# Attention, routed experts and a feed-forward network on one core: the first q and k taken by tile, and loads and weight splits handed to other engines

## The chip, the cores and the metric

The kernel runs on one core of a Trainium2 chip. The number that counts is the device time of one execution in microseconds, and the median of several runs is compared. The core has five engines with an instruction stream each, which run on their own and wait for one another on semaphores: PE (TensorE, matrix products and transposes), DVE (VectorE), ACT (ScalarE), POOL (GpSimd) and SP (SyncE, which here only issues DMA transfers). Sixteen DMA engines move the data.

## What is computed

Three stages follow one another. The numbers are `B, H, S, D = 4, 8, 576, 64`, so `N = B*S = 2304` tokens of `512` features, 8 experts of width 1024, and a last network of width 2048.

```python
# attention in a window of 64 keys
scores = scale * q @ k.T ; mask (0 <= rel < 64) ; attn = softmax(scores) ; x = attn @ v
# mixture of experts, two of eight for each token
noisy_logits = x @ w_gate + log1p(exp(x @ w_noise)) * noise
top2, top2_w = two largest, softmax over the two
for e in range(E): h = maximum(x[mask] @ w1[e], 0); out[mask] += top2_w * (h @ w2[e])
# feed-forward
h = x @ w_in ; g = h * clip(h + 3, 0, 6) / 6 ; return g @ w_out
```

## The kernel before, in words

**Attention** goes over 18 tiles of 128 tokens, `T` from 0 to 17. q and k come in chunks of two tiles, and PE turns them (`turn_qk`) so that features lie on partitions; each chunk is two *items* (`n`), one for each half of the heads. ACT moves the turned q out of PSUM (`move_first`), DVE the turned k (`move_second`). Then for each tile: `scores` on PE, `row_max` on DVE, `exps` on ACT, `transpose_p` on PE, `move_pt` on ACT, `times_v` on PE, `normalise` on DVE, which leaves the tile's output in `x_new`. PE turns this too (`transpose_x`), and multiplies it with the gates' weights `wgn` (`gate_parts`, `gate_sum`). All of it is pipelined over the tiles: iteration `T` of PE's stream holds the scores of tile `T+1`, the turning of item `T+3`, and the product with v of tile `T-1`.

**Routing** happens meanwhile in five lots of tiles, `LOTS = ((0, 3), (3, 4), (7, 4), (11, 3), (14, 4))`. For a lot, DVE works out which two experts each token goes to and its row in the sorted copy of x; the rows stand in `slot_cur`. POOL then copies `x_new` away (`keep_x`, into `x_cur`) and scatters each tile twice to the DRAM tensor `x_sorted` with an indirect DMA (`scatter(t, k)`). Experts start when the first three lots have been scattered: ACT waits for them and loads the first three blocks of expert 0 (`load_x`), and PE turns these (`turn_x`, line 1602). The last two lots are needed later in expert 0 only.

**Weights** are brought as fp32 chunks of 128x1024 into four `stage` buffers and split into a high and a low part, which PE takes as fp32r operands. An expert has `SCH = 8` chunks, four of w1 and four of w2. POOL makes both parts: `split_hi` (line 680) multiplies by one and rounds, `split_lo` (line 690) subtracts. For expert 0 this falls into attention, and each part is written in four pieces. The semaphore `w_ready` counts chunks; `hidden` of expert 0 wants four, and `project` of column block `c` wants `5 + c // 2`. A chunk's load waits until the chunk four before it is split.

**Queues.** SP issues nearly all loads in an order written out by hand: the first q (k by ACT), chunks 1 to 3 of q and k, v of tiles 0 to 2 between them, the gates' weights, and from then on, one iteration of PE after the other, v of tile `T+1`, the chunks of q and k, and the chunks of expert 0's weights where `FIRST_AT` says. v of one tile is four transfers of 64 KB. A chunk of q and k is four transfers, or six where `pieces` cuts a tile in two 64-row halves. Tables say after which tile POOL scatters (`SCATTER_AT`) and splits (`SPLIT_AT`). `pause` is a copy by POOL that nothing uses, between two scatters. Two parts of `y_sorted` are set to zero at `ZERO_AT`, the other two later.

Where POOL stands in line with the scatters of the third lot, tiles 7 to 10, the text is this:

```python
            c = len(SPLIT_AT)
            first_there(c)
            for n in range(2 * PIECES):
                if n < PIECES:
                    split_hi(0, c, PIECES, n, n + 1)
                else:
                    split_lo(0, c, c + 1, PIECES, n - PIECES, n - PIECES + 1)
                scatter(LOTS[FIRST_LOT][0] + n // 2, n % 2)
```

**After attention** PE works through eight experts and six groups of the last network without a wait of note.

## Time and profile before

| what | value |
|---|---|
| median of 3 runs | 1024.43 us (1023.0 to 1025.25) |
| profiled execution | 1019.22 us |
| its span | 1017.5 us |
| TensorE clock granted over the span | 0.991 of full |
| PE busy | 988.1 us, 97% of the span |
| DVE, ACT, POOL busy | 417.8, 227.7, 423.5 us |

The span is the stretch between the first and the last instruction of the profiled execution; 1.7 us of its time lie outside. Busy shares are averages over stages with different limits, so only views of one stretch tell what a change there is worth. PE is an engine in order: what a change saves ahead of the experts moves all that follows.

### The profile page before, as it was taken

How to read it: one execution, taken by the hardware profiler on the slowest of the kernel's cores; microseconds unless marked ns; L12 is line 12 of the kernel's file. 1: busy time of each engine (PE TensorE's matmuls, PEld its weight loads, DVE VectorE, ACT ScalarE, POOL GpSimd, SP SyncE). 2: the span in 40 equal slices, each digit the busy share in tenths (PEclk: the TensorE clock that was granted, in tenths of full speed). 3: DMA queues.
4: the chain of work that ended last, by engine and by line, in shares of the span. 5: the costliest groups of instructions: out<-in, count | busy, mean ns of one | idle time of the engine just before them, and what ended most of it. 6: DMA issues, size and time to landing. Idle time of an engine off the chain costs nothing.

```text
span 1017.5 us, 18019 instructions
## 1 busy us (share of the span) xinstructions
PE 988.1 (97%) x7108; PEld 877.5 (86%) x7108; DVE 417.8 (41%) x897; ACT 227.7 (22%) x537; POOL 423.5 (42%) x326
## 2 busy tenths in 40 slices
PE   7989889999999999999999999999999999999998
PEld 6777668989889898989989989999999999999997
DVE  3578764313222222213222255545445445355333
ACT  4666521111111111111111121111111211111111
POOL 3067976993855739192855729101101001000000
PEclk9999879999999999999999999999999999999999
DMA  9699876764452716263342433200101111000000
GB/s 181 128 207 247 271 258 222 246 186 150 135 185 90 230 61 208 70 180 122 125 145 86 151 106 125 64 32 21 42 31 41 41 31 41 31 1 1 32 1 31
DMA packets 125878, 115.94 MB, mean 114 GB/s; under 512 B 64912, under 2 KB 93520, under 8 KB 125808
## 3 DMA queue, kind: packets, MB, share of 16 engines
q1 hardware_dynamic: 106368, 75.36, 27.0%
q10 hardware_dynamic: 13680, 20.75, 6.0%
q0 software_dynamic: 5760, 18.88, 5.8%
q8 instruction: 47, 0.77, 0.3%
q14 instruction: 23, 0.19, 0.1%
HBM read 75.90 MB, written 39.06 MB: 113 GB/s over the span
## 4 chain that ended last, share of the span: by engine, by line
PE 81%; SPq 7%; POOL 5%; DMA 3%; issue 2%; DVE 1%; ACT 0%; ACTq 0%; POOLq 0%; DVEq 0%
PE PS L1635 20%; PE PS L1755 20%; PE PS L1739 19%; PE PS L1618 19%; SPq L500 3%; SPq L490 3%; POOL x_sorted L711 3%; PE PS L1602 1%; POOL W L690 1%; POOL W L680 1%; PE PS L1680 1%; DMA x_sorted<-zeros 1%; DMA y_sorted<-y_sb 0%; PE PS L1498 0%; DMA stage<-in_moe_w_dram 0%
## 5 line engine op out<-in xcount | busy, mean ns | idle before, releaser
L1635 PE MATMUL PS<-W,hs_room 128*128 128x512 f32 (+1 forms) x960 | 245.2, 399 | 0.1
L1618 PEld LDWEIGHTS PS<-xs,W 128*128 128x128 f32 x1536 | 231.0, 189 | 10.8 <-issue 0.2
L1618 PE MATMUL PS<-xs,W 128*128 128x256 f32 (+2 forms) x1536 | 239.7, 307 | 0.0
L1755 PE MATMUL PS<-W,gs 128*128 128x512 f32 x864 | 217.0, 396 | 0.9 <-DVE gs L1353 0.9
L1739 PE MATMUL PS<-x2s,W 128*128 128x384 f32 x1152 | 216.6, 337 | 0.0
L1739 PEld LDWEIGHTS PS<-x2s,W 128*128 128x128 f32 x1152 | 201.4, 188 | 7.2
L680 POOL TENSOR_TENSOR W<-stage,ones_f 128x1024 fp32r<-128x1024 f32 (+1 forms) x100 | 147.6, 1484 | 136.5 <-PE PS L1635 133.1
L1635 PEld LDWEIGHTS PS<-W,hs_room 128*128 128x128 f32 (+1 forms) x960 | 172.3, 186 | 34.6 <-DVE hs_room L1203 0.3
L1755 PEld LDWEIGHTS PS<-W,gs 128*128 128x128 f32 x864 | 161.5, 188 | 31.5 <-issue 1.6
L690 POOL TENSOR_TENSOR W<-stage,W 128x1024 fp32r<-128x1024 f32 (+1 forms) x100 | 185.4, 1863 | 5.8
L1203 DVE SCALAR_TENSOR_TENSOR hs_room<-PS,hs_room 128x256 fp32r<-128x256 f32 (+2 forms) x128 | 61.9, 484 | 290.6 <-ACT hs_room L899 290.6
L899 ACT ACTIVATE hs_room<-PS 128x256 fp32r<-128x256 f32 (+2 forms) x128 | 55.3, 432 | 371.0 <-PE PS L1618 354.2
L1012 ACT ACTIVATE gs<-PS 128x384 fp32r<-128x384 f32 x96 | 47.2, 492 | 307.6 <-DVE PS L1351 307.6
L787 POOL DMA_INDIRECT ya<-y_sorted,slot x18 | 17.1, 951 | 223.9 <-PE PS L1680 200.6
L1349 DVE TENSOR_SCALAR hc<-PS 128x384 f32<-128x384 f32 x96 | 53.5, 557 | 130.9 <-PE PS L1739 130.9
L1353 DVE SCALAR_TENSOR_TENSOR gs<-PS,gs 128x384 fp32r<-128x384 f32 x96 | 53.6, 558 | 60.5 <-ACT gs L1012 60.5
L1351 DVE SCALAR_TENSOR_TENSOR PS<-hc,PS 128x384 f32<-128x384 f32 x96 | 54.0, 562 | 3.3
L711 POOL DMA_INDIRECT x_sorted<-x_cur,slot_cur x36 | 35.7, 991 | 16.2 <-DVE slot_cur L1154 8.8
L834 ACT ACTIVATE probs<-PS,negmax 128x128 f32<-128x128 f32 x144 | 39.3, 400 | 2.9 <-DVE negmax L1068 2.9
L1216 DVE COPY y_sb<-PS 128x512 f32<-128x512 f32 (+1 forms) x40 | 27.0, 688 | 22.6 <-PE PS L1635 22.6
L1197 DVE TENSOR_TENSOR xs<-PS,xs 128x512 fp32r<-128x512 f32 (+1 forms) x40 | 27.1, 679 | 17.2 <-ACT xs L889 15.5
L718 POOL COPY x_cur<-x_new 128x512 f32<-128x512 f32 x18 | 10.9, 609 | 48.8 <-DVE x_new L1083 48.8
(133 smaller groups left out, 574.4 us busy)
## 6 DMA issues: line engine op xcount, KB each, us to landing
stage<-in_moe_w_dram SPq DMA_DIRECT2D x64, 512.0 KB, 4.2
x_sorted<-zeros SPq DMA_DIRECT2D x7, 1280.0 KB, 7.6
y_sorted<-y_sb ACTq DMA_DIRECT2D x33, 256.0 KB, 3.7
x_in<-x_sorted ACTq DMA_DIRECT2D x31, 256.0 KB, 4.3
vD<-in_v_dram SPq DMA_DIRECT2D x72, 64.0 KB, 2.8
out_dram<-o_sb SPq DMA_DIRECT2D x18, 256.0 KB, 2.1
stage<-in_moe_w_in_dram SPq DMA_DIRECT2D x8, 512.0 KB, 3.9
stage<-in_moe_w_out_dram SPq DMA_DIRECT2D x8, 512.0 KB, 3.8
```

Of the source, the lines that this page charges most:

```text
L680: last = nc.gpsimd.tensor_tensor(chunk_at(parity, c, 0)[:, at], stage[:, c % STAGES, at], ones_f[:].broadcast_to([P, n]), ALU.mult)
L690: last = nc.gpsimd.tensor_tensor(chunk_at(parity, c, 1)[:, at], stage[:, c % STAGES, at], chunk_at(parity, c, 0)[:, at].bitcast(F32), ALU. ...
L711: pool.indirect_dma_start(out=x_sorted, out_offset=bass.IndirectOffsetOnAxis(ap=slot_cur[:, k, t:t + 1], axis=0), in_=x_cur[:, t, :], in_o ...
L899: nc.scalar.activation(hs[:, c % 2, 0, 0:n], HP_[:, c % 2, 0:n], ACT.Relu).then_inc(hhi_done, 1)
L1203: nc.vector.scalar_tensor_tensor(hs[:, c % 2, 1, 0:n], HP_[:, c % 2, 0:n], 0.0, hs[:, c % 2, 0, 0:n].bitcast(F32), ALU.max, ALU.subtract). ...
L1349: nc.vector.tensor_scalar(hc[:, c % 2], h, 3.0, 0.0, ALU.add, ALU.max).then_inc(hc_done, 1)
L1351: nc.vector.scalar_tensor_tensor(G6[:, c % 2], hc[:, c % 2], 6.0, h, ALU.min, ALU.mult).then_inc(g6_done, 1)
L1353: nc.vector.scalar_tensor_tensor(gs[:, c % 2, 1], G6[:, c % 2], 1.0 / 6.0, gs[:, c % 2, 0].bitcast(F32), ALU.mult, ALU.subtract).then_inc( ...
L1618: last = nc.tensor.matmul(HP_[:, c % 2, 0:n], W[:, par, 0, b, at:at + P], xs[part][:, a, kd, 0:n], start=start, stop=(kd == KD - 1 and (a, ...
L1635: last = nc.tensor.matmul(Y[0:n, first + t, :], hs[:, c % 2, a, t * P:t * P + n], W[:, par, 1, b, c * DM:(c + 1) * DM], start=(c == 0 and ...
L1739: last = nc.tensor.matmul(H2P[:, c % 2, :], W[:, 0, kd // 2, b, at:at + P], x2s[par][:, a, kd, :], start=first, stop=(kd == KD - 1 and (a, ...
L1755: last = nc.tensor.matmul(OP[:, tt, :], gs[:, c % 2, a, tt * P:(tt + 1) * P], W[:, 1, c // FC, b, at:at + DM], start=(c == 0 and (a, b) == ...
```

## The change

Five things are done, in words of the diff:

1. **The first chunk by tiles.** The four transfers of q and the four of k of chunk 0 are issued tile by tile instead of by halves of the heads, and PE turns tile 0 (`turn_tile(0)`), computes its scores, and then turns tile 1. Item 2 goes into two other PSUM banks (`item_bank`). DVE's and ACT's first instructions are put in the same order.
2. **Fewer transfers on SP's queue.** v of tile 0 is issued by ACT; the two transfers of the gates' weights by POOL. Chunks 4 and 8 of q and k are no longer cut (SP itself adds what the semaphore lacks), so each of the two has four transfers instead of six.
3. **Three chunks ahead of the third lot.** `SPLIT_AT` keeps three chunks instead of five. The second lot's scatters end one iteration earlier, with pauses where splits stood. The fourth chunk is now the one that is split between the eight scatters of tiles 7 to 10, each scatter ahead of its piece, with two `keep_x` among them.
4. **The last two chunks** of expert 0 are split by ACT (`beside_hi`) and DVE (`beside_lo`) in expert 0 itself. `tables` and `places_in_y` move back by one column block.
5. **Loads and zeros.** The eighth chunk is issued at `T = 17` instead of 15, and there it waits for the fourth chunk's split. Three of the four zero stores of `y_sorted` stand behind it at `T = 17`. Ahead of the pads SP loads two chunks of expert 1 instead of four.

```diff
-    FIRST_AT = (4, 6, 8, 10, 12, 13, 14, 15)
-    SPLIT_AT = (7, 8, 11, 12, 13)
+    FIRST_AT = (4, 6, 8, 10, 12, 13, 14, 17)
+    SPLIT_AT = (7, 8, 11)
+    BESIDE = 2
...
-    ZERO_AT = (16, 17)
+    ZERO_AT = (16, 17, 17, 17)
...
-    SCATTER_AT = {8: 0, 9: 1, 10: 2, 12: 3, 13: 4, 14: 5, 15: 6}
+    SCATTER_AT = {8: (0,), 9: (1,), 10: (2,), 12: (3,), 13: (4, 5), 14: (6,)}
...
-                if c and c % 2 == 0 and r == (crossed or [0])[0]:
+                if r in crossed(c):
...
-            load_v(0)
+            load_v(1)
             load_qk(3, both)
-            load_v(1)
-            for n, w in enumerate((wg, wn)):
-                sp.dma_start(wgn[:, :, n * E:(n + 1) * E], w.rearrange("(k p) e -> p k e", p=P)).then_inc(s_small, 16)
             load_v(2)
...
-            load_expert(1, 0, QCH)
-            for n in range(len(ZERO_AT), ZERO_PARTS):
-                zero_y(n)
+            load_expert(1, 0, QCH - BESIDE)
...
+            for n, w in enumerate((wg, wn)):
+                nc.gpsimd.dma_start(wgn[:, :, n * E:(n + 1) * E], w.rearrange("(k p) e -> p k e", p=P)).then_inc(s_gates, 16)
...
-            for n in range(2 * PIECES):
+            for n in range(2 * LOTS[FIRST_LOT][1]):
+                scatter(LOTS[FIRST_LOT][0] + n // 2, n % 2)
                 if n < PIECES:
                     split_hi(0, c, PIECES, n, n + 1)
                 else:
                     split_lo(0, c, c + 1, PIECES, n - PIECES, n - PIECES + 1)
-                scatter(LOTS[FIRST_LOT][0] + n // 2, n % 2)
+                if n % 4 == 3:
+                    keep_x(kept)
+                    kept += 1
...
+            load_v_block(act, 0, 0)
             move_first(0)
+            load_v_block(act, 0, 1)
             move_first(1)
             exps(0)
+            move_pt(0, 0)
             move_first(2)
...
+            def beside_hi(c):
+                act.wait_ge(stage_full[c % STAGES], 16 * (c // STAGES + 1))
+                at = slice((c - QCH) * CH, (c - QCH + 1) * CH)
+                nc.scalar.copy(W[:, 0, 1, 0, at], stage[:, c % STAGES, :]).then_inc(beside_half, 1)
...
+            def beside_lo(c):
+
+                at = slice((c - QCH) * CH, (c - QCH + 1) * CH)
+                dve.wait_ge(w_ready, c)
+                dve.wait_ge(beside_half, c - (SCH - BESIDE) + 1)
+                nc.vector.tensor_tensor(W[:, 0, 1, 1, at], stage[:, c % STAGES, :], W[:, 0, 1, 0, at].bitcast(F32),
+                                        ALU.subtract).then_inc(w_ready, 1)
...
-            turn_qk(0)
-            turn_qk(1)
+            turn_tile(0)
             scores(0)
+            turn_tile(1)
             scores(1)
+            transpose_p(0, 0)
             turn_qk(2)
-            transpose_p(0, 0)
             turn_qk(AHEAD)
             transpose_p(0, 1)
```

On PE, at the start of the program, the rows before run from the turning of the first chunk (`q_raw`, `k_raw`) over the scores (`masks`, then `qkT`) of tiles 0 and 1 to item 2:

```order
L1422 MATMUL PS<-ident,q_raw 128x2x64 [waits raw_first0,s_ident]
L1422 MATMUL PS<-ident,q_raw 128x2x64 x3
L1422 MATMUL PS<-ident,k_raw 128x2x64 x4
L1422 MATMUL PS<-ident,q_raw 128x2x64 [waits raw_first1]
L1422 MATMUL PS<-ident,q_raw 128x2x64 x3
L1422 MATMUL PS<-ident,k_raw 128x2x64 x4
L1446 MATMUL PS<-masks,ident_b 64x512 [waits s_mask,ld_dve,ld_act]
...
L1461 MATMUL PS<-qkT 64x128 x16
L1422 MATMUL PS<-ident,q_raw 128x2x64 [waits sc_act,raw_full1]
```

The same place in the changed program, where the first tile's scores stand ahead of the second tile's turning:

```order
L1470 MATMUL PS<-ident,q_raw 128x128 [waits raw_first0,s_ident]
L1470 MATMUL PS<-ident,q_raw 128x128 x3
L1470 MATMUL PS<-ident,k_raw 128x128 x4
L1495 MATMUL PS<-masks,ident_b 64x512 [waits s_mask,ld_dve,ld_act]
...
L1470 MATMUL PS<-ident,q_raw 128x128 [waits raw_first1]
L1470 MATMUL PS<-ident,q_raw 128x128 x3
L1470 MATMUL PS<-ident,k_raw 128x128 x4
L1495 MATMUL PS<-masks,ident_b 64x512 [waits ld_dve,ld_act]
...
L1462 MATMUL PS<-ident,q_raw 128x2x64 [waits raw_full1]
```

The second wait for data has moved behind the first scores, and item 2 no longer waits for `sc_act`, the end of `exps(0)`.

On POOL, before, from the fourth chunk (in `stage_full3`) to the first scatters of tiles 7 to 10. A DMA row is a scatter, `x_cur<-x_new` is `keep_x`:

```order
L680 TENSOR_TENSOR W<-stage,ones_f 128x256 [waits stage_full3]
L680 TENSOR_TENSOR W<-stage,ones_f 128x256 x3
L711 DMA x_sorted<-x_cur,slot_cur 23552x512
L690 TENSOR_TENSOR W<-stage,W 128x256 [waits w_half]
L690 TENSOR_TENSOR W<-stage,W 128x256 x3
L718 COPY x_cur<-x_new 128x512 [waits out_moved]
L711 DMA x_sorted<-x_cur,slot_cur 23552x512
L680 TENSOR_TENSOR W<-stage,ones_f 128x256 [waits ld_full,stage_full0]
...
L680 TENSOR_TENSOR W<-stage,ones_f 128x256 [waits ld_full,stage_full1]
L711 DMA x_sorted<-x_cur,slot_cur 23552x512 [waits x_kept,slots_ready]
```

And in the changed program, from the last scatters of the second lot:

```order
L748 COPY idle<-x_cur 128x512 [waits paused]
L724 DMA x_sorted<-x_cur,slot_cur 23552x512
L724 DMA x_sorted<-x_cur,slot_cur 23552x512 [waits x_kept,slots_ready,stage_full3]
L693 TENSOR_TENSOR W<-stage,ones_f 128x256
L724 DMA x_sorted<-x_cur,slot_cur 23552x512
...
L693 TENSOR_TENSOR W<-stage,ones_f 128x256
L734 COPY x_cur<-x_new 128x512 [waits out_moved]
L724 DMA x_sorted<-x_cur,slot_cur 23552x512
L703 TENSOR_TENSOR W<-stage,W 128x256 [waits w_half]
```

Sixteen split rows (two chunks) are gone from in front of the scatter that waits for `slots_ready`, and that scatter now stands ahead of the first piece.

On SP, at the end of attention, before and then changed:

```order
L508 DMA stage<-in_moe_w_dram 128x2x512 [waits w_ready]
L500 DMA vD<-in_v_dram 64x4x64 [waits out_full,sc_full]
L500 DMA vD<-in_v_dram 64x4x64 x3
L513 DMA y_sorted<-zeros 1536x1x128
L513 DMA y_sorted<-zeros 2048x1x128 [waits sc_full]
L560 DMA stage<-in_moe_w_dram 128x1024 [waits x_loaded2,w_ready,x_loaded1,x_loaded0]
L560 DMA stage<-in_moe_w_dram 128x1024 [waits w_ready] x3
L513 DMA y_sorted<-zeros 2048x1x128 x2
```

```order
L488 DMA vD<-in_v_dram 64x4x64 [waits out_full,sc_full]
L488 DMA vD<-in_v_dram 64x4x64 x3
L530 DMA y_sorted<-zeros 1536x1x128
L525 DMA stage<-in_moe_w_dram 128x2x512 [waits w_ready,sc_full]
L530 DMA y_sorted<-zeros 2048x1x128 x3
L575 DMA stage<-in_moe_w_dram 128x1024 [waits x_loaded2,w_ready,x_loaded1,x_loaded0]
L575 DMA stage<-in_moe_w_dram 128x1024 [waits w_ready]
```

The last chunk of expert 0 has gone behind the last v, with a wait for `w_ready`, and three zero stores stand behind it.

## Rows read from the trace of the kernel before

**Rows 1.** The page: PE's clock and the DMA engines' share in 40 slices.
```profile
PEclk9999879999999999999999999999999999999999
DMA  9699876764452716263342433200101111000000
```

**Rows 2.** Windows: busy times, PEclk, DMA share, GB/s of two stretches.
```profile
60.00:104.00 44.00, 42.15 (x921) 33.10 (x919) 34.55 (x111) 30.10 (x90) 34.20 (x49) 1.00 0.97 234
...
132.00:143.00 11.00, 8.72 (x47) 7.66 (x48) 5.66 (x21) 2.87 (x5) 10.31 (x16) 0.55 0.66 220
```

**Rows 3.** Timeline of PE: start, duration, work, idle time before it and releaser.
```profile
9.66 0.41 PE L1446 MATMUL PS<-masks,ident_b 64*64 64x512 bf16 x4 [0.83 <-ACT qkT L828]
...
20.96 0.63 PE L1422 MATMUL PS<-ident,q_later 128*128 128x128 f32 x4 [0.23 <-ACT probs L834]
...
27.88 1.16 PE L1498 MATMUL PS<-vD,pT 64*64 64x65 f32 x64 [0.62 <-DMA vD<-in_v_dram]
...
45.21 0.63 PE L1422 MATMUL PS<-ident,q_later 128*128 128x128 f32 x4 [1.64 <-DMA k_later<-in_k_dram]
...
59.45 0.63 PE L1422 MATMUL PS<-ident,q_later 128*128 128x128 f32 x4 [1.99 <-DMA k_later<-in_k_dram]
```

**Rows 4.** Timeline of SP's DMA queue, 15 to 38 us.
```profile
15.01 3.48 SPq L500 DMA_DIRECT2D vD<-in_v_dram  x4
...
26.09 0.61 SPq L532 DMA_DIRECT2D wgn<-in_moe_w_gate_dram  x1
...
27.29 5.86 SPq L500 DMA_DIRECT2D vD<-in_v_dram  x8
...
33.99 3.30 SPq L490 DMA_DIRECT2D q_later<-in_q_dram  x3
```

**Rows 5.** Windows of 2 us near the start, columns as in rows 2.
```profile
12.00:14.00 2.00, 0.03 (x2) 0.00 (x0) 1.47 (x3) 1.69 (x7) 0.00 (x0) 1.00 1.36 208
```

**Rows 6.** Timeline of DVE, 105 to 131 us.
```profile
105.40 1.42 DVE L1130 TENSOR_TENSOR gap<-top_v 128x4 f32<-128x4 f32 x1
106.75 0.15 DVE L1076 TENSOR_SCALAR rsum<-PS 128x8 f32<-128x8 f32 x1
...
109.73 0.57 DVE L1139 TENSOR_TENSOR chosen_b<-hot 128x32 bf16<-128x32 f32 x1
...
113.75 0.16 DVE L1154 CAST slot_cur<-slot_f 128x8 int32<-128x8 f32 x1
...
128.85 2.35 DVE L1137 TENSOR_TENSOR hot<-iota_e,top_f 128x24 f32<-128x24 f32 x2
```

**Rows 7.** Timeline of POOL, 104 to 132 us.
```profile
104.01 2.78 POOL L690 TENSOR_TENSOR W<-stage,W 128x256 fp32r<-128x256 f32 x4
...
113.86 0.62 POOL L680 TENSOR_TENSOR W<-stage,ones_f 128x256 fp32r<-128x256 f32 x1
...
127.82 0.98 POOL L711 DMA_INDIRECT x_sorted<-x_cur,slot_cur  x1 [0.17 <-issue]
128.82 2.32 POOL L680 TENSOR_TENSOR W<-stage,ones_f 128x256 fp32r<-128x256 f32 x4
```

**Rows 8.** Timeline of PE, first block of expert 0.
```profile
134.55 1.12 PE L1602 MATMUL PS<-ident,x_in 128*128 128x128 f32 x4 [1.70 <-DMA x_in<-x_sorted]
```

**Rows 9.** Timeline of ACT, the load of expert 0's first blocks.
```profile
131.83 1.31 ACTq L864 DMA_DIRECT2D x_in<-x_sorted  x3
```

**Rows 10.** From issue to landing: the 36 scatters of line 711, then loads of x_in.
```profile
DMA to landing us min/median/max: 2.7/4.4/7.6
...
DMA to landing us min/median/max: 2.6/3.2/4.9
```

**Rows 11.** Line 1359, a low part made by DVE from a whole chunk.
```profile
L1359 DVE TENSOR_TENSOR W<-stage,W x4: 1215/1222/1255, 606.2 to 616.4; 128x1024 fp32r<-128x1024 f32 x4
```

**Rows 12.** Last two loads for expert 0 by SP, and PE's turning of them.
```profile
169.19 0.82 SPq L590 DMA_DIRECT2D x_in<-x_sorted  x2
...
173.13 1.04 PE L1602 MATMUL PS<-ident,x_in 128*128 128x128 f32 x8
```

115 lines of the change are left out of this document (68 added, 47 removed).

## The prediction, written before the changed kernel ran

> **What bounds the kernel now.** I read the slices of the page first. From about 150 us on the clock is full and PE has no gap, so nothing there can be won by other engines; the DMA engines are at four tenths or less from 430 us on [rows 1]. The change only touches the first 175 us. What it saves ahead of expert 0 moves the whole rest, one for one, and what it does not save there is lost. So the question is when PE turns the first block of expert 0: at 134.55 us [rows 8].
>
> Reading back from there by the timelines: PE waited 1.70 us for that block [rows 8]. ACT issued the load at 131.83 [rows 9], when the last scatter of the third lot had landed. POOL issued that scatter at 127.82 and ended it at 128.80 [rows 7], so landing took 3.0 us and the load 2.7. The eight scatters and eight pieces began at 113.86 [rows 7], which is when DVE had finished the rows of that lot, at 113.91 [rows 6]. So the end of attention hangs on **the slots of the third lot, plus a row of 15 us on POOL, plus 5.7 us of DMA**. The slots in turn hang on PE's and DVE's pace through the tiles.
>
> That pace: between 60 and 104 us PE is busy 42.15 of 44 us [rows 2]; it sets the pace itself. Ahead of 60 us it waits for loads three times: 0.62 us for v at 27.88, 1.64 for k at 45.21, 1.99 for k at 59.45 [rows 3]. SP's queue shows why. It issues without a gap: four v transfers in 3.48 us, eight more in 5.86, the three transfers of a cut chunk's q in 3.30 [rows 4]. Eight v transfers of 64 KB in 5.86 us are some 90 GB/s, half of what the DMA engines carry when they are full (208 GB/s at 12 us, rows 5). So SP's issuing, not the DMA engines, is what is late in the stretches of v.
>
> **The change, part by part.**
>
> *The start.* Before, scores of tile 0 begin at 9.66 [rows 3], after both halves are turned. By tile they can begin one turning and one move earlier, which I estimate at 1.6 us from the 0.63 us of four transposes [rows 3], twice, and a gap, the second turning lies under DVE's maxima, and item 2 does not wait for the exponentials. Worked through with the durations of these rows, item 4, at 20.96 before [rows 3], could start at about 18. That is 2.9 us, and the 0.62 wait for v goes too, because v of tile 1 is issued where v of tile 0 was. Together 3.5 us. But PE then runs into the loads at 45.21 and 59.45, which it already waits for. It keeps only what SP's queue gains.
>
> *SP's queue.* Four v transfers leave it: 8 in 5.86 us is 0.73 each [rows 4], so 2.6 to 2.9; I take 2.6, since part of the time is the wait of a full queue, which passes on to the next transfer. The gates' weights take 26.09 to 27.29, 1.2 us [rows 4]. The three transfers of the cut chunk's q took 3.30 us, 1.1 each [rows 4], so this is held by bandwidth too; two fewer of six save between 0 and 2.2, I take 0.6. Against that stand 256 KB of v, which ACT now issues early, right behind k, into DMA engines that are full: at 208 GB/s [rows 5] they push chunks 1 and 2 back by 1.2 us. Sum 2.6 + 1.2 + 0.6 - 1.2 = **3.2 us**, less than the 3.5 that the start could use. From both sides: nothing at all if the DMA engines set the pace, and 4.4 if the 1.2 us fill idle time. The Trainium skill, page "DMA: Bandwidth & Descriptors", section "Issuing engines are not separate DMA queues", says that DMAs of several engines run on the same 16 DMA engines, and that issuing from more than one saves the sequencer's time alone. Taken strictly, the v that moves to ACT would be worth its issue time of 2.6 only where the engines have room, and by it the sum would be 2.6 + 1.2 - 1.2 = 2.6. The trace has both stretches, full ones (rows 5) and ones with SP as the limit (rows 4).
>
> What the moved transfers cost their new queues: ACT issues two before its first move of q and two after; it sat idle there and is needed again only when PE's second turning ends. POOL issues two small ones while it has nothing else to do, about 1 us each by the scatters' 0.98 [rows 7], and PE wants the weights only behind the product with v at 27.88 [rows 3]. Both are costed at nothing; without that cover it is 2.6 us on ACT.
>
> *DVE's route to the slots.* At 105.40 a subtraction of four columns took 1.42 us, where an operation of eight columns right behind it took 0.15 [rows 6]. It ended when POOL's four low pieces of the fifth chunk, 104.01 to 106.79, ended [rows 7]. From 101 to 113 us I count five more operations of that route that took about 0.35 us over their like; the one at 109.73 with 0.57 us is the fourth of them [rows 6]. The change takes the fourth and fifth chunk off POOL there; the second lot's scatters end earlier as well, and POOL then waits for the slots. So the loss goes: 1.27 + 5 x 0.35 = 3.0 at most, nothing if PE is what DVE waits for. DVE's maxima wait for PE's scores in between, so I take two thirds, **2.1 us**. The Trainium skill, page "SBUF — State Buffer", section "SBUF: two separate sides", calls the pair of ports that VectorE and GpSimd share an exclusive lock, held for the whole instruction. The trace agrees, and more than one instruction deep: at 128.85 two small operations took 2.35 us and ended with POOL's four high pieces [rows 6, 7].
>
> *The row on POOL.* Before: 14.94 us from the first piece to the end of the last scatter. After: the last low piece (0.73) is behind the last scatter, one copy (0.6) is put between, and the first scatter cannot start before the slots, 0.3 after them. The row is **0.2 us longer** seen from the slots. Range 0 to 0.6.
>
> *The queue at the hand-over.* The eighth chunk's load waits for the fourth chunk's split, which ends 0.8 us behind the last scatter. So 0.5 MB of weights and 3 MB of zeros set off while that scatter lands and ACT loads x. Before, 1.75 MB of the zeros lay under the eight scatters, and the rest behind the load. The last scatter landed in 3.0 us and the first load in 2.7; medians are 4.4 and 3.2, maxima 7.6 and 4.9 [rows 10]. The last scatter has a head start, and x's own queue shares the engines with the zeros instead of standing behind them, so I take **1.0 us**, and for the range 0 to 6.8.
>
> *Expert 0.* DVE makes a low part of a whole chunk in 1.22 us [rows 11]; I take no more for a high part, a copy of the same size by ACT. PE needs some 4 us for a column block there (134.55 to 173.13 holds an opening and eight of them, rows 8 and 12), so both fit beside `h_hi` and `h_lo`; without that cover they would be 4.9 us. `project(4)` wants the seventh chunk, which is ready about 1 us ahead. Two things are tight: the loads of the last two blocks are issued from 169.19 to 170.01 and turned at 173.13 [rows 12], less than 1 us behind their landing; POOL's last eight scatters lie under DVE's two low parts. And two more chunks of expert 1 (1 MB) now come when expert 1's x is loaded. I take **0.6 us**, range 0 to 2.5.
>
> Sum: 3.2 + 2.1 - 0.2 - 1.0 - 0.6 = **3.5 us**. The first block of expert 0 is turned at about 130.5 instead of 134.55. The profiled execution would be 1015.7 instead of 1019.22 us. The median of the runs lies 5.2 us above the profiled one, and I take the difference over to it: 1024.4 - 3.5 = **1020.9 us**.
>
> **Rivals.** *(a) The DMA engines set the pace, not SP.* Their share is 0.97 from 60 to 104 us [rows 2]. If it is they who make PE wait at 45 and 59, the queue's relief gives 0.8 us instead of 3.2, and the kernel 3.5 - 2.4 = 1.1 us less, 1023.3. For it: the 1.1 us for a q transfer. Against: the v transfers at 90 GB/s, and the 6 in the second of the slices of 25 us [rows 1], which says that between 25 and 51 us the engines had room. Chance 0.19.
>
> *(b) Slower: zeros in front of x.* The hand-over hangs on one landing and one load. If the zeros take their full share, the scatter lands 4.6 us later and the load 2.3 (maxima against what they took). That is 6.9 us in place of 1.0, and the sum becomes 2.4 us slower, 1026.8. It decides from 4.5 us on. For it: a scatter took up to 7.6 us under such traffic. Against: the zeros are small packets on another ring. Chance 0.18 with its neighbours.
>
> *(c) More: the clock.* From 132 to 143 us PE ran at 0.55 of its clock on average [rows 2], after it had sat idle before 132 and again before 134.55. At 0.55 the 8.72 busy us hold about 4 us that full clock would not need. If PE comes to expert 0 with its clock up, up to 3 us more are won, 1018. I think it idles longer, since POOL's row gates it even more than now: PE should stand ready 4 us early. Chance 0.10.
>
> The forecast itself has 0.53. The measurement tells about 0.2%, 2 us, from no change. Faster by more takes the forecast but for its slow edge, (c), and a piece of (a): 0.62. Within 2 us: most of (a) and the edge of (b): 0.20. Slower: (b), 0.18. The range reaches from (c) with the start's 4.4, 1015.5, to just beyond (b), 1027.5.
>
> **What the profile would show.** PE's waits at 45.21 and 59.45 stay but come 3 us earlier; if they are gone, SP won more. Scores of tile 0 begin near 8 us. The slots of the third lot are ready near 108.5, with no DVE operation of 1.4 us ahead of them. The last scatter of that lot ends near 123.5. The first load of x is issued 3 to 3.5 us later and lands in 3 to 4; PE's wait ahead of its first block (line 1602 before) grows from 1.70 to about 5. If the scatter or the load takes over 6 us there, (b) is at work. Wrong altogether would be a wait of PE for `w_ready` in expert 0, or one ahead of the last two blocks or of expert 1.

## The result and the profile after

The changed kernel takes **1027.41 us** (median of 22 runs, 1023.05 to 1031.68) against 1024.68 us for the kernel before (22 runs, 1018.67 to 1028.2) on the same chip: the ratio is **1.0029, 95% interval 1.0015 to 1.0043**. It is 2.7 to 3 us slower. The forecast was 3.5 us faster.

One thing first about the profiles. The profiled execution of before, 1019.22 us, was 5.5 us under the median of its runs; that of the changed kernel, 1028.67, is 1.3 over. So the two spans (1017.5 and 1026.6) overstate the difference threefold, and what separates them from 60 to 104 us is mostly not the change, as e13 and e14 show below. Differences between kernels are taken from ratios, and the profiles are read for mechanisms.

Windows of the changed kernel, columns as in [rows 2]:
```profile
60.00:104.00 44.00, 38.77 (x848) 29.74 (x852) 30.81 (x103) 28.15 (x85) 30.88 (x43) 1.00 0.98 239
...
170.00:200.00 30.00, 27.62 (x161) 24.40 (x161) 11.00 (x30) 5.23 (x11) 25.61 (x14) 0.94 0.85 279
```
The second stretch was whole before, and this is its line there:
```profile
170.00:200.00 30.00, 29.90 (x189) 26.64 (x188) 9.37 (x18) 6.22 (x14) 29.45 (x15) 1.00 0.85 263
```
Between 170 and 200 us PE was busy all but 0.1 us, at a granted clock of 1.00. Now it idles for 2.4 us, and its clock falls to 0.94 on average.

The start, on PE's timeline, against [rows 3]:
```profile
7.47 0.41 PE L1495 MATMUL PS<-masks,ident_b 64*64 64x512 bf16 x4 [0.83 <-ACT qkT L851]
...
14.26 0.66 PE L1462 MATMUL PS<-ident,q_raw 128*128 128x128 f32 x4 [1.55 <-DMA k_raw<-in_k_dram]
...
20.93 0.66 PE L1462 MATMUL PS<-ident,q_later 128*128 128x128 f32 x4 [2.47 <-DMA k_later<-in_k_dram]
...
57.55 0.63 PE L1462 MATMUL PS<-ident,q_later 128*128 128x128 f32 x4
```
Scores of tile 0 begin at 7.47, 2.2 us earlier, and the gain is gone at 20.93, before's 20.96: PE waits for k of chunks 1 and 2. It comes back further on: the waits for k that before had at 45.21 and 59.45 are gone, and the item it turned at 59.45 is turned at 57.55. SP's queue, against [rows 4]:
```profile
16.40 3.93 SPq L488 DMA_DIRECT2D vD<-in_v_dram  x4
...
23.95 6.99 SPq L488 DMA_DIRECT2D vD<-in_v_dram  x8
31.07 1.49 SPq L565 DMA_DIRECT2D x_sorted<-zeros  x1
32.66 2.46 SPq L508 DMA_DIRECT2D q_later<-in_q_dram  x2
```
Chunk 4 is issued 1.3 us earlier (33.99 before), not 3.2: the same eight v transfers now take 6.99 us instead of 5.86.

The hand-over to expert 0, lines of POOL, SP, ACT and PE put together in order of time, against [rows 7 to 9]:
```profile
116.51 0.97 POOL L724 DMA_INDIRECT x_sorted<-x_cur,slot_cur  x1 [8.26 <-issue]
130.07 0.98 POOL L724 DMA_INDIRECT x_sorted<-x_cur,slot_cur  x1 [0.17 <-issue]
131.90 0.38 SPq L525 DMA_DIRECT2D stage<-in_moe_w_dram  x1
132.32 10.02 SPq L530 DMA_DIRECT2D y_sorted<-zeros  x3
132.90 1.90 ACTq L891 DMA_DIRECT2D x_in<-x_sorted  x3
139.10 1.11 PE L1651 MATMUL PS<-ident,x_in 128*128 128x128 f32 x4 [2.21 <-DMA x_in<-x_sorted]
```
The last transfer of the third lot ends at 131.05 and has landed at 132.90, after 1.9 us (3.0 before). The load of x issued then needs 6.2 us to reach PE (2.7 before): 0.5 MB of weights and the first of three zero stores of 1 MB were issued 1.0 and 0.6 us ahead of it. The second store was issued with it, at 132.94, and the third at 137.09.

The hand-over to expert 1, in the same way:
```profile
176.66 0.57 SPq L591 DMA_DIRECT2D x_sorted<-zeros  x1
177.28 16.99 SPq L575 DMA_DIRECT2D stage<-in_moe_w_dram  x6
183.71 1.35 ACTq L891 DMA_DIRECT2D x_in<-x_sorted  x3
189.17 1.05 PE L1651 MATMUL PS<-ident,x_in 128*128 128x128 f32 x4 [2.38 <-DMA x_in<-x_sorted]
189.87 2.91 PE L1684 MATMUL PS<-W,hs_room 128*128 128x512 f32 x6
```
The same place before:
```profile
170.78 0.57 SPq L576 DMA_DIRECT2D x_sorted<-zeros  x1
...
177.79 1.40 ACTq L864 DMA_DIRECT2D x_in<-x_sorted  x3
...
181.74 0.60 PE L1602 MATMUL PS<-ident,x_in 128*128 128x128 f32 x4
```
In the changed kernel the padding is issued at 176.66 and loads of weights follow at once, two of them into free buffers. The x load comes 7.0 us behind the padding, as before, and lands 5.5 us later; PE waits 2.38 us, and its next six matmuls take 2.91 us, where the same group took 1.56 us at 183.82. Before had no wait there. A wait of PE ahead of expert 1 is one of the three things that the prediction had named as "wrong altogether".

### The profile page after: what moved, and what is told of

Same layout as the page of the kernel before. It is cut to its first block, busy times and chain, and to the rows that moved or that the text cites. A ratio compares the mean times of both kernels' runs of the same rounds, so it can differ in the third digit from the quotient of the medians.

```text
span 1026.6 us, 18010 instructions
## 1 busy us (share of the span) xinstructions
PE 993.1 (97%) x7108; PEld 879.6 (86%) x7108; DVE 415.5 (40%) x899; ACT 230.7 (22%) x539; POOL 419.0 (41%) x315
## 4 chain that ended last, share of the span: by engine, by line
PE 83%; POOL 4%; issue 3%; DMA 3%; SPq 3%; DVE 2%; ACT 0%; POOLq 0%; DVEq 0%; ACTq 0%
PE PS L1804 19%; PE PS L1684 19%; PE PS L1788 19%; PE PS L1667 19%; POOL x_sorted L724 2%; SPq L508 2%; PE PS L1651 2%; PE PS L1547 1%; POOL W L703 1%; PE PS L1729 1%; PE PS L1526 1%; SPq L488 1%; POOL W L693 1%; DMA x_sorted<-zeros 1%; PE PS L1510 1%
## 5 line engine op out<-in xcount | busy, mean ns | idle before, releaser
L693 POOL TENSOR_TENSOR W<-stage,ones_f 128x1024 fp32r<-128x1024 f32 (+1 forms) x92 | 143.1, 1562 | 137.9 <-PE PS L1684 134.4
L703 POOL TENSOR_TENSOR W<-stage,W 128x1024 fp32r<-128x1024 f32 (+1 forms) x92 | 180.1, 1965 | 5.7
```

Source lines behind the costliest of these rows:

```text
L693: last = nc.gpsimd.tensor_tensor(chunk_at(parity, c, 0)[:, at], stage[:, c % STAGES, at], ones_f[:].broadcast_to([P, n]), ALU.mult)
L703: last = nc.gpsimd.tensor_tensor(chunk_at(parity, c, 1)[:, at], stage[:, c % STAGES, at], chunk_at(parity, c, 0)[:, at].bitcast(F32), ALU. ...
```

## The experiments

The series of runs differ in level. The kernel before had medians of 1024.5 (e1 to e4), 1019.4 (e5 to e8), 1024.1 (e9 to e12), 1019.6 (e13 to e16) and 1018.3 us (e17, e18). The second and the third series have the same chip number on record, 7, so the level isn't the chip's alone. Every ratio is to the runs of before in its own series. The ratios on record are not quotients of the two medians, and differ from them most in e3 and e10, whose medians alone would give 0.9999 and 1.0002. "Late" means behind the load that it stood ahead of.

| kernel | ratio | its series' before |
|---|---|---|
| changed | 1.0029; 1.0046; 1.0026 | 1024.7; 1024.1; 1019.6 |
| e1, e15 front part only | 0.9981; 0.9983 | 1024.5; 1019.6 |
| e7 by tile only | 1.0004 | 1019.4 |
| e2 back part only | 1.0069 | 1024.5 |
| e3, e17 zeros late | 1.0015; 1.0012 | 1024.5; 1018.3 |
| e4 expert 1's loads ahead of the padding | 1.0036 | 1024.5 |
| e10, e18 expert 1's loads late | 1.0024; 1.0008 | 1024.1; 1018.3 |
| e5, e16 both late | 0.9980; 0.9976 | 1019.4; 1019.6 |
| e6 back part only, both late | 1.0016 | 1019.4 |
| e11 both late, transfers first | 1.0007 | 1024.1 |
| e12 front part, transfers first | 1.0042 | 1024.1 |
| e8, e13 before again | 0.9997; 1.0002 | 1019.4; 1019.6 |

### e1 and e2: the two halves of the change

e1 is before with the first chunk by tile and the moves on the queues (V0 to ACT, the gates' weights to POOL, uncut chunks). e2 is before with the rest: the constants, POOL's order, the two chunks by ACT and DVE, the late loads of expert 1. In the cut below e1's lines are against the changed kernel and e2's against the kernel before.
```
 e1:  -    FIRST_AT = (4, 6, 8, 10, 12, 13, 14, 17)   e2:  +    FIRST_AT = (4, 6, 8, 10, 12, 13, 14, 17)
      +    FIRST_AT = (4, 6, 8, 10, 12, 13, 14, 15)        +    SPLIT_AT = (7, 8, 11)
           ... all of before's back part                   +    BESIDE = 2 ... all of before's start
```


> The kernel before with points 1 and 2 of the change alone (first chunk by tile, v of tile 0 by ACT, gates' weights by POOL, uncut chunks 4 and 8). Theory A, the loss is made at the hand-over and in expert 1's loads: this kernel is 0 to 2 us faster than before, and PE turns item 4 near 21 us as before, since v pushed chunk 2 back. Rival B, the start itself costs (PE idles ahead of item 4, its clock falls, later tiles find the DMA queues fuller and stall): 1 to 4 us slower, with PE's clock below 1.00 between 20 and 26 us and the turning of item 17 later than in the kernel before (102.64 us).

> The kernel before with points 3 to 5 alone (three chunks ahead of the third lot, the last two by ACT and DVE, eighth chunk and zeros at tile 17, two instead of four chunks of expert 1 ahead of the pads). Theory A: slower than before by 2 to 6 us, PE's first block of expert 0 later than 134.55 us by 0 to 4 and a wait of over 1 us ahead of expert 1's first block. Rival B: within 1 us of before or faster by up to 2, since the slots come earlier without POOL's splits.

Measured (with the 95% interval of the ratio, here and below): e1 1021.72 us, **0.9981** (0.9964 to 0.9998). e2 1032.0 us, **1.0069** (1.0046 to 1.0092). The front is a gain of 2 us and the back a loss of 7; both together are less bad than the back alone by more than the front is worth. In e2 the x load of expert 1 came late, and PE stood still for 5.45 us. Lines of SP, DVE, PE and ACT, in order of time:
```profile
176.02 0.57 SPq L580 DMA_DIRECT2D x_sorted<-zeros  x1
177.04 2.48 DVE L1303 TENSOR_TENSOR moved<-moved,blk 128x252 f32<-128x252 f32 x1
...
184.23 0.54 DVE L1219 SCALAR_TENSOR_TENSOR hs_room<-PS,hs_room 128x368 fp32r<-128x368 f32 x1
184.83 4.21 PE L1662 MATMUL PS<-W,hs_room 128*128 128x512 f32 x9 [5.45 <-DVE hs_room L1219]
...
190.93 1.39 ACTq L873 DMA_DIRECT2D x_in<-x_sorted  x3
```
From padding to load it is 14.9 us here, 7.0 in the changed kernel. What held it was DVE. ACT made a high part about 1.8 us late, behind POOL's last transfers (the last section has this), so DVE came to the nine small operations of `places_in_y` and the last routing part at 175.17, when POOL's splits had begun (174.63). They took 9.0 us. In the changed kernel they ran from 172.91 to 175.4, ahead of POOL's splits at 175.27, and took 2.5; `moved` took 0.42 us there and 2.48 here. The low part `h_lo` that PE wanted stood behind them, and ACT issues the x load behind its next high part. So a part of e2's loss is this chain and not the loads, and e6, in a series without ACT's late start, doesn't have it.

### e3 and e4: one transfer moved

e3 puts the last three stores of zeros where before had two of them, behind the first x loads. e4 loads expert 1's first four chunks ahead of the padding, as before.
```
 e3:  -    ZERO_AT = (16, 17, 17, 17)
      +    ZERO_AT = (16,)
       ...
           load_expert(1, 0, QCH - BESIDE)
      +    for n in range(len(ZERO_AT), ZERO_PARTS):
      +        zero_y(n)
 e4:  -    load_expert(1, 0, QCH - BESIDE)
      +    load_expert(1, 0, QCH)
           ... and load_expert(1, QCH) behind the padding
```


> The changed kernel with the three zero stores of tile 17 put behind expert 0's loads and the first two chunks of expert 1. Theory A: the load of expert 0's first block lands in about 3 us instead of 6.2, and the kernel is 2 to 3.5 us faster than the changed one, near before. Rival B: PE's wait for that block shrinks but the time stays within 1 us of the changed kernel, since something else (DVE's logits, the scatters) is as late.

> The changed kernel with all four w1 chunks of expert 1 loaded ahead of the pads, as before the change. Theory A: PE's wait of 2.38 us ahead of expert 1's first block and the low clock behind it go, 2 to 4 us faster than the changed kernel. Rival B: the third and fourth chunk wait for the splits of the last two chunks of expert 0, hold up the pads and the last two blocks of expert 0, and PE waits there instead: no gain or up to 4 us slower.

Measured: e3 1024.47 us, **1.0015** (0.9996 to 1.0033). e4 1027.48 us, **1.0036** (1.0022 to 1.005). In e4 the third of the four loads waits for a free buffer, which DVE's last low parts give back (21.2 us; the four take 26.7 us in SP's queue), and the padding and x of expert 0's last two blocks wait behind it: PE waits 2.38 us at 180.39 for these blocks. The wait ahead of expert 1's first block is gone (turned at 189.39); PE waits 1.19 us for DVE behind it, at 191.23. The wait has only moved. Moving loads ahead is no cure, since their buffers come free late.

### e5 and e6: both transfers late

SP also waits until expert 1's first three blocks of x have landed. e6 is e2 with the same two moves.
```
       pad(1, 1, 0)
 +     sp.wait_ge(x_loaded[PARTS[0][1] - 1], 32)
       load_expert(1, QCH - BESIDE)
```


> The changed kernel with its last three stores of zeros put late, as in e3, and in addition SP waits until the first three blocks of expert 1's x have landed before it issues the last six chunk loads of expert 1 (two of which find a free buffer at once). Theory H, the two hand-overs: beside the zeros it is the 1 MB of weights set off in front of expert 1's x that costs, PE's 2.1 us at 184.80 in e3 and the slow clock behind it, about 3.5 us in all. Then the median falls from e3's 1024.5 to about 1021 (0.9965 to 0.998 of before), x of expert 1 lands in 3 to 4 us instead of 6 to 7, and PE has no wait ahead of expert 1's first block. Theory R, the row on POOL: what is left of the loss sits ahead of 140 us, in the later slots and in DVE's maxima behind POOL's pieces. Then it stays within 1 us of e3 (1.000 to 1.0015), even if that wait is gone.

> The kernel before with points 3 to 5 of the change alone (as e2), the three stores of zeros put late and expert 1's last six chunk loads behind its x. Theory H (the two queues are all that is bad in the back part): e2's 1032.0 loses 3 for the zeros and the 5.45 us wait ahead of expert 1 with some of its slow clock, 8 us in all, 1024 (0.998 to 1.001 of before). Theory R (the row on POOL itself costs): 1027 to 1029 (1.0025 to 1.0045), with expert 0's first block turned 2 us or more later than before's 134.55.

Measured: e5 1017.17 us, **0.998** (0.9968 to 0.9992). e6 1020.2 us, **1.0016** (1.0001 to 1.0031). With both late the whole change is as good as the front part. The back part alone, with both late, is still 0.2% slow, at or just over the upper end of what theory H gave it, and its twelve runs scatter over 8 us; the reason stays open.

### e7: by tile alone

```
       load_qk(1, both)
       load_qk(2, both)
 -     load_v(1)
 +     load_v(0)
       load_qk(3, both)
 +     load_v(1)
 +     ... wgn by SP
       load_v(2)
       ... chunks 4 and 8 cut, and all of before's back part
```
The lines are against the changed kernel.


> The kernel before with q and k of the first chunk by tile, and nothing else: v of tile 0, the gates' weights and the cut chunks stay as they were, all on SP. Theory S (the prediction's: the start's gain is caught by the loads that SP issues late): PE waits at chunk 4 and 5 stay or grow by what the start won, and the median is within 1 us of before (0.999 to 1.000). Theory T (the start itself carries it): as e1, 0.998.

Measured: 1019.62 us, **1.0004** (0.9994 to 1.0014), nothing. PE's timeline shows before's waits in place:
```profile
44.98 0.63 PE L1430 MATMUL PS<-ident,q_later 128*128 128x128 f32 x4 [0.75 <-DMA k_later<-in_k_dram]
...
59.03 0.63 PE L1430 MATMUL PS<-ident,q_later 128*128 128x128 f32 x4 [1.92 <-DMA k_later<-in_k_dram]
```
So the start's own gain is caught by late loads, as forecast, and e1's 2 us come only with the moves on the queues. The moves without the start by tile were not run, so whether they need it isn't shown.

### e8, e9 and e10: before again, changed again, loads late alone

e8 and e9 change nothing. e10 is the changed kernel with e5's wait of SP and the zeros where the change has them.

> The kernel before, unchanged, as a second look. Its ratio should be 1.000 within 0.002, which gives the size of what such a comparison cannot tell. Its first profile (1019.2 us) lies 5 us under its median (1024.5); a second should lie nearer. Theory C (the stalls called issue of about 1 us inside the product with v at 72 to 76 and 94 to 103 us, which every changed kernel shows and the first profile of before does not, belong to the program): they are missing here too. Theory I (they come and go with the execution, whatever the kernel): one or both stand here, and item 17 is turned at 104 or later instead of 102.64.

> The changed kernel, unchanged, measured beside the next three and again beside the kernel before, for a profile that stands on the same footing as theirs. Its ratio to before should be 1.003 within 0.002 again. Theory I (the stalls called issue and the 4.5 us lost between 60 and 104 us come with the execution, as their absence in the last four profiles suggests): PE is busy 41 us or more of these 44. Theory C (they come with the changed program): 39 or less.

> The changed kernel with its zeros where it has them, and only the last six chunk loads of expert 1 put behind the landing of that expert's x. It completes the square: changed 1.0029, zeros late 1.0015, both late 0.998. Theory H (two costs that add up): about 0.9995, since the loads were worth 0.0035. Theory O (they overlap: with the zeros in front expert 0 starts late and the rest has slack, or the reverse): 1.001 or more. The first load of expert 0's x still lands 5.5 to 6.2 us behind its issue and PE has no wait of over 0.5 us for x of expert 1.

Measured: e8 1018.58 us, 0.9997 (0.9985 to 1.001). e9 1027.67 us, 1.0046 (1.0027 to 1.0065). e10 1024.26 us, 1.0024 (0.9997 to 1.0051), too wide to tell. Neither e8 nor e5 to e7 have stalls called issue inside the product with v from 70 to 105 us; e9 to e12 all have them. e9's PE was busy 40.1 of the 44 us, between what the two theories asked for. That left open whether the stalls go with the series; e13 to e18 bear on it.

### e11 and e12: POOL's transfers ahead of its pieces

```
 -     first_there(c)
       for n in range(2 * LOTS[FIRST_LOT][1]):
           scatter(LOTS[FIRST_LOT][0] + n // 2, n % 2)
 -         split_hi or split_lo of piece n
       ...
 +     first_there(c)
 +     split_hi(0, c, PIECES)
 +     split_lo(0, c, c + 1, PIECES)
```


> Both late, and on POOL the eight transfers of the third lot stand ahead of the fourth chunk's eight pieces instead of between them, so that the pieces lie beside the last landing and the load of x. Theory P (POOL's row sets the end of attention, as the prediction has it): eight transfers at 1.27 us take 10.2 us instead of 14.5, the last one ends near 121 instead of 125.2, and x of expert 0 could be turned 3 to 4 us earlier; PE itself is only free at 126.3, so the first block moves from 130.45 to about 127 and the kernel wins 3 us, 0.995 of before. Theory D (the DMA engines write the rows no faster than they are now sent, or chunk 4's pieces, which then end near 127.3, are waited for by the hidden layer): the landing grows by what the row shrinks, and the ratio stays at 0.998.

> The front part of the change alone (as e1, 0.998), with POOL's eight transfers of the third lot ahead of the fourth chunk's eight pieces. Theory P: 2 to 3 us less than e1, 0.995 to 0.996. Theory D: as e1. Against e11 it says what the rest of the back part (two chunks taken by ACT and DVE, one transfer pair moved) is worth once the order of the row is right: nothing by the profile so far, and then both are equal.

Measured: e11 1023.8 us, **1.0007** (0.9986 to 1.0028). e12 1027.4 us, **1.0042** (1.0019 to 1.0064). In e11 one copy, `keep_x`, still stands between the fourth and the fifth transfer; in e12 nothing does. Both theories missed. The row did shrink, to 10.4 us (115.08 to 125.47), but DVE stood still for it. DVE's timeline, and PE's behind it, in e11:
```profile
116.57 0.16 DVE L1195 TENSOR_TENSOR gate<-gap 128x4 f32<-128x4 f32 x1
125.34 0.69 DVE L1102 TENSOR_REDUCE negmax<-PS 128x4 f32<-128x512 f32 x1 [8.62 <-remote]
...
127.01 1.08 PE L1559 MATMUL PS<-ident,x_new 128*128 128x128 f32 x4 [9.12 <-DVE logits L1126]
```
PE had ended the scores that these maxima read 8.5 us earlier, at 116.82. DVE started them when POOL was in its last transfer (124.50 to 125.47). In e12 the same place has 8.42 us.

### e13 to e16: four kernels in one series

No code is new: before, changed, front part, both late.

> The kernel before, unchanged, a third look, in one series of runs with the changed kernel, its front part and both late. The series differ: before had a median of 1024.5, 1019.4 and 1024.1 us in the three so far, and the stalls that the profile calls issue and remote stood in every profile of the first and third and in none of the second. Theory I (the stalls belong to the series, not to the program): if before lies near 1024 here, the stalls of about 1 us inside the product with v at 70 to 105 us stand in this profile too, and PE is busy 40 us or less of 60 to 104 us; if it lies near 1019, they are missing in all four. Theory C (they belong to the change): a series near 1024, and none here.

> The changed kernel, unchanged, beside the three others of this series. Ratio to before 1.003 to 1.0045 as twice before. If the series is one near 1019, DVE's late start of the maxima of tile 17 (1.6 us behind POOL's second transfer, called remote) is missing, and what is left of the loss is the two hand-overs: PE waits of 2 us at 139 and at 189. Theory H (the hand-overs carry it): still 1.003. Theory R (the DVE stall under POOL's row carries it): 1.000 to 1.001 in such a series.

> The front part alone, again, beside both late. Its first ratio was 0.9981 in a series near 1024. If the front part's gain is SP's queue, it holds in any series: 0.997 to 0.999. If it was chance, 1.000.

> The whole change with the zeros and expert 1's loads out of the way of the two landings, again, beside the front part and the changed kernel. Its 0.998 came from the series near 1019. Theory H: it stays at 0.998 in any series, equal to the front part alone, so the rest of the back part is worth nothing and costs nothing. Theory R: in a series near 1024 the row on POOL stalls DVE and it falls to 1.000 or above, while the front part alone keeps 0.998.

Measured: e13 1019.22 us, 1.0002 (0.9991 to 1.0014). e14 1022.08 us, **1.0026** (1.0013 to 1.0039). e15 1017.73 us, **0.9983** (0.9972 to 0.9995). e16 1017.16 us, **0.9976** (0.9964 to 0.9988). The ratios are those of theory H: the series is one near 1019, DVE's late start at tile 17 is missing in e14, and the loss is there all the same. Moving the zeros and six loads takes 5 us off the changed kernel. One reserve goes with this: e14's profiled execution took 1017.18 us, the fastest of its twelve and 1.7 us less than e13's (1018.89). So the loss of 2.6 us is in the ratio, and no profile of this series shows it whole.

The turning of expert 0's first block, before (e13), changed (e14) and both late (e16), one line of PE's timeline from each:
```profile
135.16 1.12 PE L1602 MATMUL PS<-ident,x_in 128*128 128x128 f32 x4 [5.86 <-DMA x_in<-x_sorted]
```
```profile
132.01 1.12 PE L1651 MATMUL PS<-ident,x_in 128*128 128x128 f32 x4 [6.21 <-DMA x_in<-x_sorted]
...
180.06 0.66 PE L1651 MATMUL PS<-ident,x_in 128*128 128x128 f32 x4 [2.05 <-DMA x_in<-x_sorted]
```
```profile
131.62 1.12 PE L1653 MATMUL PS<-ident,x_in 128*128 128x128 f32 x4 [4.79 <-DMA x_in<-x_sorted]
```
In this series before is ready for the block long before it comes (it waits 5.86 us), so POOL's row alone decides. The changed kernel is 3.1 us ahead there, a microsecond less than the 4.1 that the forecast had for this point (130.5 for 134.55). Of these it has 0.6 left when expert 1's first block is turned (180.06; before turned it at 180.62, without a wait).

Two stretches, put beside each other for the profiles, show where the loss sits. The first is from the end of the third lot's last transfer to PE's turning of expert 0's first block. The second is from the turning of expert 0's last two blocks to that of expert 1's last two (172.01 to 215.62 in e13). With it stands PE's busy time from 170 to 200 us.

| profile | first, us | second, us | PE busy, clock 170:200 |
|---|---|---|---|
| before: e8, e13 | 4.6, 6.0 | 43.5, 43.6 | 29.8, 29.7; 1.00 |
| front: e1, e15 | 6.1, 5.9 | 43.9, 44.0 | 29.4, 29.2; 1.00 |
| both late: e5, e16 | 5.2, 5.3 | 44.1, 44.3 | 29.6, 29.6; 1.00 |
| zeros late: e3, e17 | 7.6, 5.2 | 45.6, 47.1 | 27.9, 27.8; 1.00, 0.94 |
| loads late: e10, e18 | 8.1, 6.9 | 44.8, 44.0 | 29.6, 29.6; 1.00 |
| changed: first, e9, e14 | 8.1, 8.2, 6.7 | 47.4, 47.3, 45.6 | 27.6, 27.5, 28.0; 0.94, 0.94, 1.00 |

The first profile of before has 5.8 and 43.4. The second column splits the kernels without overlap: 43.4 to 44.8 us where no loads stand ahead of expert 1's x, 45.6 to 47.4 where the loads do. The first column depends on the series too (e1, e3, e10, e9 and the first changed profile are from those near 1024); in the series near 1019 it is 5.2 to 5.3 with the zeros late and 6.7 to 6.9 with them in front. Before itself has 4.6 to 6.0 there, so a difference from before of under about 1.4 us says little in this column.

### e17 and e18: each late alone, in one series

> The changed kernel with its last three stores of zeros late and expert 1's loads where the change has them, again. It stood at 1.0015 where the kernel before had 1024.5 us; changed and both late were 1.0026 and 0.9976 where before had 1019.6. Theory H, two costs that add up: about 1.000 in a series near 1019, halfway. Theory K (a cost is paid mostly through TensorE's clock, when PE's idle time at a hand-over is followed by half speed, so what counts is which of the waits is still there): with the wait ahead of expert 1's x left in place, it stays nearer the changed kernel, 1.001 or more.

> The changed kernel with the last six loads of expert 1 behind that expert's x, and the zeros where the change has them, again. It stood at 1.0024 (0.9997 to 1.0051) where before had 1024.1 us. Theory H: about 1.000, as its counterpart. Theory K: PE stands idle at the first hand-over in the kernel before as well (5.9 us in its last profile) and is at half speed behind it in any case, so the zeros cost only their delay, and the loads are the larger part: 0.999 or less here, 1.001 or more for the counterpart.

Measured: e17 1019.73 us, **1.0012** (0.9997 to 1.0028). e18 1019.13 us, **1.0008** (0.9999 to 1.0017). Theory H's halfway, within the intervals. Of theory K, e17 reached the bound and e18 did not (0.999 or less was asked). From the changed kernel's 1.0026, zeros late take 1.4 us, loads late 1.8, both 5.1; that both together take 1.9 more than the sum is within the errors (each ratio is known to about 1 to 1.5 us, and the two pairs are from different series), and a share for each beyond "about equal" is not to be had from these runs.

## Why the prediction was wrong, step by step

**The start and SP's queue (3.2 us): right in kind, too large.** The start's own gain is caught by loads (e7: nothing), the moves on the queues carry it. At item 17 the front part was 2.8 us ahead of before (100.89 in e15, 103.69 in e13), but before's own profiles have that item at 101.29 (e8), 102.64 and 103.69, so one pair of profiles is a weak scale. At expert 0's first block it was 1.8 us ahead (133.35), and by ratio it is worth 1.7 to 1.9 us. What was over-counted is the relief of SP: with four v transfers moved to ACT, the eight behind them take longer (6.6 to 7.0 us in e14, e1, e15 and the changed kernel, for 5.9 and 6.2 in before and e13), which the sum had only as the 0.3 us between its 2.9 and 2.6 and as the 1.2 us of the full stretch. One of PE's two waits for k is also still there in e15 (2.18 us at 57.83). That is rival (a), in part. Windows of the changed kernel at the start and under those eight v transfers:
```profile
2.00:18.00 16.00, 11.69 (x156) 10.17 (x159) 5.58 (x12) 7.46 (x19) 9.57 (x26) 1.00 1.27 204
24.00:31.00 7.00, 7.00 (x150) 5.63 (x144) 3.95 (x10) 5.10 (x17) 0.61 (x1) 0.90 0.71 139
```
Up to 18 us the DMA engines' share is over 1 (1.15 in before) and the rate is nearly before's (204 and 201 GB/s), so transfers issued sooner only queue there; under the v transfers the share is 0.71 and SP is still slower. The first of these agrees with the Trainium skill, "DMA: Bandwidth & Descriptors", section "Issuing engines are not separate DMA queues": issuing from a second engine saves the sequencer's time alone. By it the prediction had 2.6 us; measured were under 2.

**DVE's route to the slots (2.1 us): right in size, as far as single profiles tell.** The operation that took 1.42 us at 105.40 took 0.17 in the changed kernel; but it took 0.41 and 0.18 in before's other two profiles, so the term's largest item was in part that execution's. The slots were ready 4.3 us earlier than before in one series (110.02 and 114.32), 1.9 of which the front part has by itself (112.46). So the back part gives 2.4. Over all profiles near 1019 the whole change, with or without its late transfers, has the slots at 109.2 to 111.0 (five profiles), and before at 111.7 to 114.3 (three).

**The row on POOL (-0.2 us): right.** It takes 15.3 us from the slots to the end of the last transfer in e14, 14.9 in e13, so 0.4 longer. The last one ended 3.9 us earlier than before (125.33 and 129.21). Over the same five and three profiles it ended at 125.5 and 128.8 on average, 3.3 us earlier.

**The queue at the hand-over (-1.0 us): the first step that failed.** The prediction let the zeros slow the landing of the last transfer and the load by 1 us together. The landing did not grow: 1.9 to 2.5 us in the three profiles of the changed kernel, where before's three have 1.9 (e8), 3.0 and 3.2. The zeros wait for the fourth chunk's split and were issued 0.6 to 1.3 us ahead of the end of that landing. All of it fell on the load of x: issue to turning 4.8 us (e14) to 6.2 (changed) for 2.7 to 2.8. Seen from the last transfer the stretch is 0.7 to 2.3 us longer than in before, and 1.4 and 1.7 us longer than with the zeros late (e14 and e16, e18 and e17). Against before's 4.6 in e8 even the zeros late are 0.6 us longer, so the pairs with the zeros late are the firmer measure. Rival (b) named this mechanism, with a decision point at 4.5 us and a price of 6.9; it was never that large, and it would not have turned the sign alone.

**Expert 0 and 1 (-0.6 us): the second, and the larger miss.** "Two more chunks of expert 1 now come when expert 1's x is loaded" was seen, and priced at 0.6 with 2.5 as its worst. Against before's 43.5 us the stretch around it is 2.1 us longer in e3 and e14, and 3.6 to 3.9 in e17, e9 and the changed kernel's first profile. PE's wait itself is 2.12 and 2.05 us in these two, and 2.22, 2.52 and 2.38 in the other three. So in two profiles the stretch grew by the wait alone, and in three by 1.3 to 1.5 us more; these three are the ones whose clock fell. Windows of 4 us around that wait, e9, where the first holds the wait's start:
```profile
184.00:188.00 4.00, 2.79 (x18) 2.30 (x17) 0.04 (x1) 0.31 (x1) 2.67 (x2) 1.00 1.04 404
188.00:192.00 4.00, 2.70 (x9) 2.31 (x10) 1.54 (x3) 1.05 (x3) 3.92 (x3) 0.61 1.05 364
```
The granted clock is 0.61 on average in the second, between full speed (2.4 GHz) and half (1.2). The same place in e14:
```profile
176.00:180.00 4.00, 2.01 (x15) 1.71 (x13) 0.85 (x2) 0.77 (x2) 3.65 (x2) 1.00 1.04 390
180.00:184.00 4.00, 3.94 (x25) 3.58 (x26) 0.71 (x2) 0.97 (x2) 3.92 (x3) 1.00 1.02 344
```
Here the clock stays at 1.00. Of the five profiles in the table that have both the loads in front and the wait, three show the fall (changed, e9, e17), e3 and e14 do not; what decides it isn't shown. The prediction had only asked what the clock could give, in rival (c), and not what a new wait costs in a stretch that had no gap. The estimate of 2.5 for the worst case had the length of the wait and not what follows it.

**Where the sum ends.** Ahead of the first hand-over most of the forecast stood: 3.3 to 3.9 us are gained by the last transfer of the third lot, where its first three steps make 5.1. The two hand-overs take 5.1 by ratio (1.0026 against 0.9976), where it had 1.6. With the 3.9 that leaves 1.2 us of loss, of the 2.6 measured in that series. The rest was lost between the hand-overs, or isn't explained: e16's first block is turned 3.5 us earlier than before's, its last two only 1.7 (170.34 and 172.01). From 132 to 140 us its granted clock was 0.50 and 0.51 in windows of 4 us, where before had 0.50 and 0.67, so an earlier start is in part paid at half speed. The range held the time, by 0.1 us and in part by luck: rival (b)'s 1026.8 lies 0.6 us from the measured time, but its mechanism gave 0.7 to 2.3 of its 6.9 us, and what filled the sum was a wait that no rival had. The likeliest case, with its sign, was wrong. The lower end, 1015.5, is also lower than its own terms make it: 3.5, 1.2 for the start and 3 for the clock are 7.7, which gives 1016.7.

**Open.** e14's profile is 4.9 us under the median of its twelve runs; a typical one of the changed kernel in that series is not seen. What makes the back part alone, with both late, slower than before (e6) isn't settled either.

## What to carry to other kernels

A transfer that nobody waits for still has a place in the queue: ask of each one moved which landing is the next that an engine waits for, and put it behind that. Here three stores of zeros put behind a load of x, and a wait of SP for the landing of the next, which itself does nothing, turned 0.26% slower into 0.24% faster (e14 and e16), while issuing the same loads earlier only moved the wait (e4). Where a bottleneck engine has no gap, price a new wait with the clock behind it: waits of 2.1 to 2.5 us made the stretch 2.1 to 3.9 us longer. And compare profiles only within one series; a profile 5 us under its own median, set against one above it, showed a difference three times the true one.

## What the runs showed of the hardware

**Stalls that go with the series.** In every profile of a changed or partly changed kernel from the series whose before was near 1024, PE stopped for 0.2 to 0.7 us inside or behind the product with v ("issue") several times between 70 and 105 us, and was busy 38.8 to 40.4 of the 44 us from 60 to 104. In every profile of the series near 1019, before's or not, these stops are missing and it is 41.0 to 42.6. The windows of e13 and e14:
```profile
60.00:104.00 44.00, 42.56 (x915) 33.63 (x914) 33.18 (x108) 29.85 (x89) 33.71 (x49) 0.96 0.97 230
```
```profile
60.00:104.00 44.00, 42.23 (x968) 33.11 (x959) 35.53 (x114) 29.86 (x90) 33.30 (x46) 1.00 1.04 252
```
The changed kernel has 38.77 and 40.14 us in two series and 42.23 in the third, though in an execution 4.9 us under its median; e5, e16 and e18, which hold all of the change's code for attention and whose profiles lie within 0.2 us of their medians or above them, have 42.38, 41.70 and 41.94. So the stops aren't the change's. The one profile of before beside such a series is the first, of an execution 5 us under its median, and it has none of them (42.15 us busy). So that the kernel before has them too when it takes 1024 us is likely, since its median moves by 5 us with the series as the others' do, but not shown. What they are is not settled.

**DVE held while POOL issues indirect transfers in a row.** With eight of them in a row DVE did nothing for 8.6 us (e11) and 8.4 (e12), with its input from PE ready for nearly all of it in e11, and went on about when the last one ended (125.47 and 128.58; DVE at 125.34 and 128.75). With a piece of the split between two transfers the late start was 1.6 to 1.8 us (changed kernel, e2, e3, e4, e9, e10), and in the series near 1019 there was none. The profile names no engine as the releaser ("remote"). e1, e2 and e12 have a like late start on ACT, over POOL's last eight transfers: ACT sat idle for 5.4 us where 3.6 is usual there, and went on 1.8 us after PE had ended what it waited for, 1.4 to 1.6 us behind the last transfer (174.13 in e2). In the kernel before a copy that nobody reads stands between the two transfers of a tile in the second lot. That such a copy keeps DVE going was not tried by itself, and one instruction between is not enough: in e11 POOL made a copy at 119.88, behind the fourth transfer, and DVE stood still through it.
